# Attention and two gated layers on one core: value products on half the array's rows

## What is computed

```python
scores = scale * np.matmul(q, k.transpose(0, 1, 3, 2))
scores = cap * np.tanh(scores / cap)
attn = np.exp(scores - max); attn = attn / sum(attn)
x = np.matmul(attn, v)                       # heads side by side: 1792 x 768
h = np.maximum(np.maximum(x @ w1, x @ w2), x @ w3)
x = h @ w_out                                # 768 wide
g = x @ w_gate; val = x @ w_val              # 1536 wide
out = (g * sigmoid(g) * val) @ w_out2
```

## Time and profile before

| what | value |
|---|---|
| median of 3 runs | 992.5 us (990.97, 992.5, 997.14) |
| the profiled execution | 990.72 us, its span 988.9 us |
| granted TensorE clock | 1.0 of the full rate throughout |
| TensorE busy / weight loads | 981.1 us / 822.2 us |
| DVE, ACT, POOL busy | 745.9, 530.8, 650.3 us |

### The profile page before, as it was taken

One profiled execution on the slowest core, in us unless ns is written; L12 is line 12 of the kernel. 1 busy time (PEld: TensorE's weight loads), 2 busy tenths in 40 slices (PEclk: granted clock), 3 DMA queues, 4 the chain that ended last, 5 costly groups with the idle time before them and its releaser, 6 DMA issues. The chain is left out here.

```text
span 988.9 us, 14171 instructions
## 1 busy us (share of the span) xinstructions
PE 981.1 (99%) x4678; PEld 822.2 (83%) x4678; DVE 745.9 (75%) x938; ACT 530.8 (54%) x950; POOL 650.3 (66%) x592
## 2 busy tenths in 40 slices
PE   9999999999999999999999999999999999999998
PEld 5555555569999999999999999999999999999997
DVE  5999999983867798885378896657589888238884
ACT  7899998853433455544355454334355554335540
POOL 4568889788998567656466486565475765656651
PEclk9999999999999999999999999999999999999999
DMA  7899998998755333335533885333333333643345
GB/s 224 258 294 299 296 292 278 307 310 264 218 173 171 102 112 112 108 109 154 174 112 105 298 279 168 106 112 105 103 116 94 118 107 92 197 142 109 108 146 174
DMA packets 125800, 174.16 MB, mean 176 GB/s; under 512 B 14240, under 2 KB 122656, under 8 KB 125728
## 3 DMA queue, kind: packets, MB, share of 16 engines
q1 hardware_dynamic: 125728, 173.26, 56.5%
HBM read 133.79 MB, written 39.42 MB: 175 GB/s over the span
## 5 line engine op out<-in xcount | busy, mean ns | idle before, releaser
L632 POOL TENSOR_TENSOR w_lo<-whole,w_hi 128x384 fp32r<-128x384 f32 x420 | 473.6, 1152 | 254.7 <-ACT w_hi L800 254.7
L741 PE MATMUL acc<-a_hi,w_hi 128*128 128x448 f32 x882 | 323.2, 366 | 0.3
L741 PE MATMUL acc<-a_hi,w_lo 128*128 128x448 f32 x882 | 322.8, 366 | 0.0
L741 PE MATMUL acc<-a_lo,w_hi 128*128 128x448 f32 x882 | 322.7, 366 | 0.0
L800 ACT ACTIVATE w_hi<-whole 128x384 fp32r<-128x384 f32 x420 | 201.2, 515 | 73.1 <-DMA whole<-w_in 42.8
L741 PEld LDWEIGHTS acc<-a_hi,w_hi 128*128 128x128 f32 x882 | 165.6, 188 | 16.3 <-ACT p L822 0.9
L741 PEld LDWEIGHTS acc<-a_lo,w_hi 128*128 128x128 f32 x882 | 165.6, 188 | 14.1
L741 PEld LDWEIGHTS acc<-a_hi,w_lo 128*128 128x128 f32 x882 | 165.6, 188 | 13.9
L813 ACT ACTIVATE b_hi<-b_whole 128x448 fp32r<-128x448 f32 x126 | 70.5, 575 | 158.8 <-DVE b_whole L1012 65.8
L693 PE MATMUL acc<-prob,v_one 128*128 128x448 f32 (+1 forms) x384 | 141.8, 559 | 0.5 <-ACT prob L795 0.2
L597 POOL TENSOR_TENSOR raw_w<-raw_w 128x384 f32<-128x384 f32 x96 | 102.6, 1069 | 56.9 <-DMA raw_w<-w_in 51.3
(11 more groups left out here) (74 smaller groups left out, 990.7 us busy)
## 6 DMA issues: line engine op xcount, KB each, us to landing
whole<-s_store SPq DMA_DIRECT2D x240, 192.0 KB, 2.4
whole<-w_in SPq DMA_DIRECT2D x180, 192.0 KB, 2.4
raw_w<-w_in SPq DMA_DIRECT2D x24, 768.0 KB, 6.7
s_store<-raw_w SPq DMA_DIRECT2D x24, 768.0 KB, 8.3
qk_raw<-qk_in SPq DMA_DIRECT2D x23, 480.0 KB, 5.7
part_store<-sig SPq DMA_DIRECT2D x24, 224.0 KB, 3.0
sig<-part_store SPq DMA_DIRECT2D x24, 224.0 KB, 3.6
out<-sig SPq DMA_DIRECT2D x24, 224.0 KB, 2.9
```

Of the source, the lines that this page charges most:

```text
L632: nc.gpsimd.tensor_tensor(w_lo[:, n % RING, :], whole[:, n % RING, :], w_hi[:, n % RING, :].bitcast(F32), ALU.subtract).then_inc(w_lo_done, 1)
L741: last = nc.tensor.matmul(bank(q, BANK_OF[i]), w[:, n % RING, cols], m[:, i, c, :], start=(i < 4 and c == 0 and t == 0), stop=(c == KCH - ...
```

## The change

Each full value product of 128 keys becomes two products of 64 keys. For every step there are a first kind (head 0 on rows 0 to 63, head 1 on rows 64 to 127) and a last kind (head 0 on rows 64 to 127, head 1 on rows 0 to 63). The two products of a kind use the two halves of the array's rows and write two banks. The kinds write the same banks from other rows, so that each kind waits for the other: a new semaphore `half_done` counts first kinds. The mixed step has only a last kind; its keys change sides (head 0 now on rows 64 to 127), in the keys, the values and the products. On TensorE the first kinds stand behind the even score step, the last kinds behind the odd one.

```diff
-            def values(a):
+            def value_of_head(a, h, half, start, stop):
+                g, c = divmod(a, CH)
+                rows = slice(half * REST, (half + 1) * REST)
+                first, n = (V_MIXED + h * HEAD_DIM, 0) if c == CH - 1 else (c * 2 * P + h * P, h)
+                return nc.tensor.matmul(value_banks(g)[:, h, 0:SEQ], v_one[rows, g % NV, first:first + P],
+                                        prob[rows, a % NP, n, :], start=start, stop=stop)
+
+            def values_first(a):
                 g, c = divmod(a, CH)
                 if c == 0:
                     pe.wait_ge(v_loaded[g % NV], 32 * (g // NV + 1))
                     if g >= 2:
                         pe.wait_ge(norm_done, g - 1)
+                elif c % 2 == 0:
+                    pe.wait_ge(value_done, a)
                 pe.wait_ge(exp_done, a + 1)
-                for h in range(2):
-                    if c == CH - 1:
-                        rows, first, n = slice(h * REST, (h + 1) * REST), V_MIXED + h * HEAD_DIM, 0
-                    else:
-                        rows, first, n = slice(0, P), c * 2 * P + h * P, h
-                    last = nc.tensor.matmul(value_banks(g)[:, h, 0:SEQ], v_one[rows, g % NV, first:first + P],
-                                            prob[rows, a % NP, n, :], start=(c == 0), stop=(c == CH - 1))
-                last.then_inc(value_done, 1)
+                value_of_head(a, 0, 0, c == 0, False)
+                value_of_head(a, 1, 1, c == 0, False).then_inc(half_done, 1)
+
+            def values_last(a):
+                g, c = divmod(a, CH)
+                if c % 2 == 0:
+                    pe.wait_ge(half_done, 3 * g + min(c + 2, 3))
+                else:
+                    pe.wait_ge(exp_done, a + 1)
+                value_of_head(a, 0, 1, False, c == CH - 1)
+                value_of_head(a, 1, 0, False, c == CH - 1).then_inc(value_done, 1)
...
-            values(0)
+            values_first(0)
             scores(3)
-            values(1)
+            values_first(1)
+            values_last(0)
+            values_last(1)
             for a in range(2, STEPS, 2):
                 if a + 2 < STEPS:
                     scores(a + 2)
+                values_first(a)
+                if (a + 1) % CH < CH - 1:
+                    values_first(a + 1)
+                if a + 2 < STEPS:
                     scores(a + 3)
-                values(a)
-                values(a + 1)
+                values_last(a)
+                values_last(a + 1)
...
-        last[:, 0, :, 0] = pairs(a)[:, 0, 3 * KEYS:].transpose(0, 2, 1)
-        last[:, 1, :, 1] = pairs(a)[:, 1, 3 * KEYS:].transpose(0, 2, 1)
+        last[:, 0, :, 1] = pairs(a)[:, 0, 3 * KEYS:].transpose(0, 2, 1)
+        last[:, 1, :, 0] = pairs(a)[:, 1, 3 * KEYS:].transpose(0, 2, 1)
...
-        last = pairs(a)[:, :, 3 * KEYS:].reshape(ALL_PAIRS, P, HEAD_DIM)
+        last = pairs(a)[:, ::-1, 3 * KEYS:].reshape(ALL_PAIRS, P, HEAD_DIM)
```

More of the change, by code:

```diff
@@ L274, in build @@
         exp_done = sem("exp_done")
+        half_done = sem("half_done")
         value_done = sem("value_done")
```

## The result

| | before | changed |
|---|---|---|
| median | 993.59 us (12 runs, 985.4 to 1002.9 but for one of 2490) | 1001.56 us (12 runs, 992.8 to 1002.5 but for one of 1197 at a granted clock of 0.75) |
| ratio of the runs, 95% interval | | 1.0099 (1.0068 to 1.013) |
| profiled execution, span | 990.72 us, 988.9 us | 1002.51 us, 1000.7 us |

I had forecast 991.3 us within 985 to 1001 and a fall of 1.2 us; the kernel came out about 1% slower.

A forecast was written before the change was run, and what follows sets the result against it. TensorE's own stream was taken to set the first 15 pairs' pace (8.49 us each), DVE next. DVE's waits -2.4 and the end +1.2 gave -1.2 us on a median of 992.5: 991.3 us, range 985 to 1001.

The forecast's parts named there:

- TensorE's period: Attention, time per pair of heads: 8.49 us becomes 8.70 in ten pairs with a weight cast, 8.29 in thirteen.
- Switches: TensorE changing between 64-row and 128-row products: about 0.195 us each, two of four per pair go, 9.4 us in all.
- halves overlap in long groups: TensorE's value products: four 64-row products take as long as two of 128 rows, 4 passes of 0.375 us.
- the loop through ACT: Attention, tanh to exp on ACT, then TensorE to the next tanh: 8.70 us with a weight cast, 8.29 without.
- Little look-ahead: Rival, value products: a weight load of 0.19 us lies open at three places per pair; 998.8 us; chance 0.12.
- products in turn: Rival, value products: each of a pair's four value groups ends 0.375 us late, 9.60 us per pair; 1020 us; chance 0.10.
- the time that I drew from the page's rule: Mixed value step on TensorE: matmuls strictly in program order would need 1.66 us, where the trace has 1.02.
- The end: Attention's end, from TensorE's wait for DVE's multiply to the later stream: 6.83 us instead of 5.63, 1.2 us more.
- DVE's gain of 2.4 us: DVE in the attention: its waits for value products, 2.0 us and at most 3.4 with gaps, vanish; taken as 2.4.
- The sum's last step: Later TensorE stream, from 213.5 us, taken as untouched: the -1.2 us at its beginning carries to the kernel's end.

The follow-up runs named there:

- e3: Changed kernel with ACT's weight cast moved behind the exp of step c = 1 instead of c = 0: 1000.45 us, ratio 1.0064.
- e4: Changed kernel with both score steps ahead of both kinds of value products, as before the change: 996.99 us, ratio 1.0053.
- e1: Changed kernel run again, nothing edited: 1000.56 us, ratio 1.0085.
- e2: Changed kernel with POOL waiting once, before its low part of weight block 20, for DVE's first maximum of product group 1: 999.97 us, ratio 1.0056.
- g2: Changed kernel with the later stream's first matmul repeated 15 times in front of that stream: 1003.27 us, ratio 1.012.
- i1: Changed kernel a third time, nothing edited, in another job: 992.31 us, ratio 0.9998.
- f3: Kernel before run again, nothing edited, for a second trace: 997.63 us, single run.
- g1: Kernel before with the later stream's first matmul repeated 15 times (3.0 us on TensorE): 996.28 us, ratio 1.0039.
- f2: Changed kernel with POOL's early weight sums almost left out and their loads and stores cut to 64 of 384 columns: 991.68 us, ratio 0.9986.
- f4: Kernel before with ACT's weight cast moved behind the exp of step c = 1: 995.6 us, ratio 0.9991.
- g3: Kernel before with score and value steps interleaved one by one in the new order, value products still of 128 rows: 991.44 us, ratio 1.0014.
- h2: Kernel before with the last pair's mixed score step moved between its first two value steps: 987.57 us, ratio 0.9972.
- h1: Changed kernel with the last pair's mixed score step moved ahead of its first kinds, nothing else: 992.77 us, ratio 0.9979.
- i2: Same kernel as h1 (last mixed score step early), in one job with i1: 996.99 us, ratio 1.0009.
- f1: Kernel before with POOL's early weight sums almost left out and their loads and stores cut to 64 of 384 columns: 990.85 us, ratio 0.998.
- g4: Changed kernel with ACT's weight cast behind c = 1 and the last pair's mixed score step ahead of its first kinds: 992.54 us, ratio 1.0022.
- h3: Same kernel as g4 (cast moved, last mixed score step early), in another job: 993.43 us, ratio 0.998.

## Why the prediction was wrong

**TensorE's period: right.** Switches cost what I read off, halves overlap in long groups, the loop through ACT closes with 8.70 and 8.30 us (e3 takes the cast out of it, e4 trades it for 0.34 us waits). Little look-ahead (8.67 and 8.89) and products in turn (9.6) are out by the period. So is the time that I drew from the page's rule that matmuls start strictly in the program's order (the Trainium skill, "TensorE: Matmul & The Clock Gate", Part 3, The mechanism): eight 64-row passes lie within 1.77 us. Whether the rule itself fails here stays open. I had taken head 0's two passes to stand ahead of head 1's, and the trace doesn't show the order in which they were queued.

**The end: right, a little small.** 7.25 - 5.73 = 1.5 us more; I had 1.2. In the other traces of the changed attention it takes 7.25 (e1), 7.37 (e2, g2) and 7.67 us (i1), and 5.73 again in f3 and g1: 1.65 us more in the mean, inside my bounds of 1.0 to 2.2.

**DVE's gain of 2.4 us: wrong.** This is the step that gave the forecast its sign. From DVE's reciprocal of pair 0 to that of pair 21 the kernel before took 185.5 us, the changed one 205.10 - 18.36 = 186.7. Its recorded work is the same: 176.1 us before, and after

```profile
18.40:205.12 186.72, 176.23 (x159) 1.00 0.90 287
```

What changed in this pair of traces are its waits (total, times, longest, in the same stretch):

```profile
DVE qk_hi L939 <- DMA qk_raw<-qk_in: 5.2, 6, 1.4
DVE sums L957 <- PE acc L689: 1.1, 2, 0.8
```

It waited 0.9 us less for value products and 2.0 us more for the loads of queries and keys. I had taken the second for given. One pair of traces makes this look too firm, however. The same stretch in all traces of the two attentions, between the same two reciprocals:

| trace | stretch, us | waits for value products | waits for loads | DVE's recorded work |
|---|---|---|---|---|
| before | 185.48 | 2.0 | 3.2 | 176.1 |
| f3 | 185.36 | 2.1 | 4.5 | 174.7 |
| g1 | 185.46 | 2.1 | 4.4 | 174.9 |
| changed | 186.74 | 1.1 | 5.2 | 176.3 |
| e1 | 187.19 | 0.9 | 5.4 | 176.8 |
| e2 | 185.98 | 1.4 | 5.7 | 174.7 |
| g2 | 183.83 | 1.5 | 3.7 | 174.4 |
| i1 | 181.54 | 1.3 | 4.3 | 171.7 |

In the mean the change takes 0.8 us from the waits for value products, adds 0.8 us to those for loads (the kernel before has 4.5 itself in f3), and the stretch is 0.4 us shorter, not 2.4. The term was mis-sized by 2.0 us: I had counted on the whole wait for value products and the gaps around it, but 1.2 of its 2.0 us stay, and what is won goes to the waits for loads. The spread is larger than either figure, 5.6 us in the changed kernel, and comes mostly from DVE's own instructions: its work ranges from 171.7 to 176.8 us. That DMA engines had a share of 0.90 in this stretch stood in the earlier trace rows, and I did not read it as a bound. Whether traffic or the order on SP makes the loads late was not separated. f2 takes away traffic and POOL's sums together.

**What the attention costs in the end.** Stream starts of five traces with the changed attention: 216.6, 218.0, 216.2, 213.9, 212.3, mean 215.4; of three with the attention of before: 213.5, 213.5, 214.1, mean 213.7. So about +1.7 us, with a spread of 6 us in the one and half a microsecond in the other, where I had -1.2: the end +1.65, the first pair +0.4, DVE's stretch -0.4. The first pair I had not costed (first reciprocal 18.4 against 18.0, in the means 18.7 against 18.3). With POOL and DMA cut the sum is +1.3. The 1.7 isn't clear of the noise: full products with one step or cast moved start the stream at 215.6 (f4), 214.5 (g3) and 215.3 (h2). Only the end's part is, since the three traces of before agree on it to 0.01 us.

**The sum's last step: the part that missed the size.** I wrote that the later stream is not touched and carried the shift to the end. The code is untouched, but its pace is not a constant: from first to last matmul the stream took 766.7 us in h2 and 781.0 in e3, 14.3 us apart at a granted clock of 1.0. Of the 8 us between the medians about 1.7 (in the profiled pair 3.1) come from the attention. The rest lies in the stream. In the profiled pair most of that is the standstill, which e1 doesn't have; in the other slow traces it is the slower pace for more of the time. That this holds for the untraced runs is likely and not shown. Whether the change makes the slower pace more likely stays open. For it: three jobs at 1.0085 to 1.012 (the last with 0.3% added), and 22 of 24 runs of the changed kernel over 997 us in the first two, where 8 of the 35 runs of before beside e1 are. Against it: i1 at 0.9998 with the same instructions and 3 of 12 runs over 997 us; h1, with the same products and order but for one step, at 0.9979; and no trace in which an event of the attention could be followed to where the pace changes. Tried and not the cause: the long DVE instruction (e1), the place of the last score step (h2, i1), and, less firmly, the later start (g1).

No version tried beats the kernel before beyond its interval.

## What to carry to other kernels

Split products on halves of the array cost no array time and save a switch of 0.195 us each, but two kinds that add to one bank need a wait, and what is put in its place to hide it can close a loop through the engine that feeds the products: add up that loop, it was right here to 0.01 us. Where three engines and the DMA are all 90% busy or more, a gain on one is worth what the next one's waits allow, its DMA waits too. And before a change of 1% is forecast or believed, look at how the largest stretch that it doesn't touch varies between executions, and repeat the comparison on another job: here one kernel gave 1.0099 and 0.9998.

## What the runs showed of the hardware

**Two paces of one matmul stream.** Stretches of 100 us at a granted clock of 1.00 hold 493 to 496 matmuls or 485 to 486. The recorded length tells them apart as well, least, median and greatest of a line in h2 (fast throughout) and in e3 (slow throughout):

```profile
L741 PE MATMUL acc<-b_hi,w_lo x378: 362/365/369, 330.7 to 982.0; 128*128 128x448 f32 x189
```

```profile
L757 PE MATMUL acc<-b_hi,w_lo x378: 367/368/368, 331.6 to 995.0; 128*128 128x448 f32 x189
```

The pace holds for hundreds of microseconds. In eight of the twenty traces it fell at a stop of 0.45 to 0.48 us from start to start: at 376 to 382 us (e1, e2, e4, f3, i1) or at 761 to 763 us (before, f4, i2). In three it fell within 1 us of a hole of 0.02 to 0.05 us (f1, g4, h3, 571 to 578 us), and in two, the changed kernel's at 622 us and h1's at 614 us, no wait stands beside it. So a stop is neither needed nor enough: g1 and h2 stop at 381 and 379 us and stay fast. Behind the fall no wait of over 0.1 us followed until the end: e1 stops for the last time at 381 us, e3 never. The changed kernel's trace began at the slower pace and went on at the faster one behind its standstill (147 matmuls from 220 to 250 us, 150 from 265 to 295). What sets the pace stays open.

**A DVE instruction kept waiting for 14 us.** With two operands in SBUF it started 30 ns before an instruction of POOL (238.24), and ended at 252.40, 0.5 us behind the last of POOL's unbroken row of 14 instructions (250.88 + 1.04 = 251.92). The same instruction took 0.90 us before, beside the same kind of row. Seen once in the traces; that POOL kept DVE waiting is the likely reading, and e2, where it took 1.50 us, can't prove it.

**Clock.** Behind the standstill of 4.4 us matmuls took 0.37 us from start to start, the 1.2 GHz level, for some 3 us; the stops of 0.46 us from start to start (some 0.26 us of hole) brought no such thing.
